# Second weight tile loaded by ScalarE's queue, the first in two parts, three warm-up products in place of four

## The reference

```python
def reference(**kwargs):
    ...
    attn_out = _attn_ref(**attn_kwargs)                 # blocks of 64, a decaying state
    x = ...                                             # 1536 x 512
    x = _moe_ref(x=x, **moe_kwargs)                     # leaky relu between w_in and w_out
    return _moe2_ref(x=x, **moe2_kwargs)

def _moe2_ref(x, w1, w2, w3, w_out):
    a = x @ w1
    b = x @ w2
    h = a * b @ w3
    return (h @ w_out).astype(np.float32)
```

## Time and profile before

| | us |
|---|---|
| median of 3 runs | 512.49 (512.42 to 512.62) |
| the profiled execution | 512.28 |
| its span, first to last instruction | 510.4 |
| TensorE (PE) busy | 505.6 |
| VectorE (DVE) busy | 355.2 |
| ScalarE (ACT) busy | 200.8 |
| GpSimd (POOL) busy | 93.2 |

### The profile page before, as it was taken

One profiled execution on the slowest core, in us unless ns is written; L12 is line 12 of the kernel. 1 busy time (PEld: TensorE's weight loads), 2 busy tenths in 40 slices (PEclk: granted clock), 3 DMA queues, 4 the chain that ended last, 5 costly groups with the idle time before them and its releaser, 6 DMA issues.

```text
span 510.4 us, 9091 instructions
## 1 busy us (share of the span) xinstructions
PE 505.6 (99%) x3568; PEld 417.5 (82%) x3568; DVE 355.2 (70%) x537; ACT 200.8 (39%) x356; POOL 93.2 (18%) x101
## 2 busy tenths in 40 slices
PE   8999999999999999999999999999999999999997
PEld 6888888888888888888888888888888888888886
DVE  4667356767786876877665777697777755878962
ACT  5364243343556433333311546443333214473420
POOL 2223132111122311333300020323333300000000
PEclk9999999999999999999999999999999999999999
DMA  8999582534121111111000031212221116240012
GB/s 278 345 393 334 170 297 85 159 125 127 42 84 42 42 41 42 42 42 41 5 38 0 22 83 34 77 52 88 57 89 63 41 43 205 82 166 0 13 50 103
DMA packets 27065, 51.57 MB, mean 101 GB/s; under 512 B 4232, under 2 KB 4496, under 8 KB 27024
## 3 DMA queue, kind: packets, MB, share of 16 engines
q1 hardware_dynamic: 24560, 43.53, 25.7%
q10 hardware_dynamic: 2432, 7.47, 4.4%
q0 software_dynamic: 32, 0.00, 0.0%
HBM read 45.74 MB, written 5.25 MB: 100 GB/s over the span
## 4 chain that ended last, share of the span: by engine, by line
PE 99%; DVE 0%; issue 0%; DVEq 0%
PE acc L1438 12%; PE acc L1440 11%; PE acc L1439 11%; PE hid L1639 10%; PE hid L1638 10%; PE hid L1637 10%; PE hid L1438 7%; PE hid L1439 7%; PE hid L1440 7%; PE hid L1467 1%; PE hid L1482 1%; PE hid L1495 1%; PE acc L1764 1%; PE acc L1763 1%; PE acc L1765 1%; PE hid L1506 1%
## 5 line engine op out<-in xcount | busy, mean ns | idle before, releaser
L1438 PE MATMUL acc<-g_hi,wb 128*128 128x512 f32 x224 | 87.6, 391 | 0.0
L1439 PE MATMUL acc<-g_lo,wb 128*128 128x512 f32 x224 | 87.2, 389 | 0.0
L1440 PE MATMUL acc<-g_hi,wb 128*128 128x512 f32 x224 | 87.2, 389 | 0.0
L710 POOL TENSOR_TENSOR w_in_lo_place<-stage 128x256 f32<-128x256 f32 x16 | 12.6, 788 | 211.6 <-PE hid L1639 121.7
L1438 PE MATMUL hid<-xy_hi,wa_hi 128*128 128x512 f32 x128 | 50.3, 393 | 0.0
L1440 PE MATMUL hid<-xy_hi,wa_lo 128*128 128x512 f32 x128 | 49.8, 389 | 0.0
L1439 PE MATMUL hid<-xy_lo,wa_hi 128*128 128x512 f32 x128 | 49.8, 389 | 0.0
L1637 PE MATMUL hid<-wa_hi 128*128 128x512 f32 x128 | 49.8, 389 | 0.0
L1638 PE MATMUL hid<-wa_lo,wa_hi 128*128 128x512 f32 x128 | 49.8, 389 | 0.0
L1639 PE MATMUL hid<-wa_hi,wa_lo 128*128 128x512 f32 x128 | 49.8, 389 | 0.0
L1438 PEld LDWEIGHTS acc<-g_hi,wb 128*128 128x128 f32 x224 | 42.0, 188 | 8.9
(11 more groups left out here) (222 smaller groups left out, 931.1 us busy)
## 6 DMA issues: line engine op xcount, KB each, us to landing
stage<-weights SPq DMA_DIRECT2D x109, 256.0 KB, 3.0
w_out_place<-attn ACTq DMA_DIRECT2D x12, 512.0 KB, 4.9
x_hi_place<-attn SPq DMA_DIRECT2D x4, 512.0 KB, 8.9
w_out_place<-attn SPq DMA_DIRECT2D x4, 512.0 KB, 7.8
w_dram<-x_lo_place SPq DMA_DIRECT2D x8, 256.0 KB, 4.4
stage<-w_dram SPq DMA_DIRECT2D x8, 256.0 KB, 2.7
x_lo_place<-attn SPq DMA_DIRECT2D x2, 512.0 KB, 6.5
x_hi_place<-attn ACTq DMA_DIRECT2D x2, 512.0 KB, 6.4
```

Source lines behind the costliest of these rows:

```text
L710: nc.gpsimd.tensor_tensor(s_1, a21, a22, ALU.add).then_inc(s_made, 1)
L1438: nc.tensor.matmul(out, w_hi, a_hi, start=first, stop=False)
L1439: nc.tensor.matmul(out, w_hi, a_lo, start=False, stop=False)
L1440: return nc.tensor.matmul(out, w_lo, a_hi, start=False, stop=final)
```

## The change

The warm-up has three products. SyncE loads the first tile, w3's, in two parts: 128 columns (the left side of the first matmul) with a semaphore of their own, `first_loaded`, then the other 384. The second tile, wl's, is issued by ScalarE before lam's load. ScalarE rounds the first part, then the second tile (both count in `first_hi_done`), then the rest of the first tile, which adds 2 to `hi_done`. TensorE's first matmul waits for `first_hi_done`, its second for `hi_done`. VectorE waits for `first_hi_done` ahead of its first split.

```diff
-WARM_UP = 4
+WARM_UP = 3
...
-            for w in range(8):
+
+            first = source_of(ORDER[0])
+            sp.dma_start(stage[:, STAGED[0], 0:P], weights[first][:, 0:P]).then_inc(first_loaded, 16)
+            sp.dma_start(stage[:, STAGED[0], P:TOK], weights[first][:, P:TOK]).then_inc(staged[STAGED[0]], 16)
+            for w in range(2, 8):
                 load_weight(w)
...
         def _(act):
+            act.dma_start(stage[:, STAGED[1], :], weights[source_of(ORDER[1])]).then_inc(staged[STAGED[1]], 16)
             act.dma_start(pow_row[:, BLOCK:BLOCK + 1], lam).then_inc(lam_loaded, 16)
...
-            w = 0
-            for _ in EARLY_34:
+
+            w3_hi, wl_hi = dest(ORDER[0])[0], dest(ORDER[1])[0]
+            act.wait_ge(first_loaded, 16)
+            nc.scalar.copy(w3_hi[:, 0:P], stage[:, STAGED[0], 0:P]).then_inc(first_hi_done, 1)
+            act.wait_ge(staged[STAGED[1]], 16)
+            nc.scalar.copy(wl_hi, stage[:, STAGED[1], :]).then_inc(first_hi_done, 1)
+            act.wait_ge(staged[STAGED[0]], 16)
+            nc.scalar.copy(w3_hi[:, P:TOK], stage[:, STAGED[0], P:TOK]).then_inc(hi_done, 2)
+            w = 2
+            for _ in EARLY_34[2:]:
                 weight_hi(w)
                 w += 1
...
+            dve.wait_ge(first_hi_done, 2)
             for w in range(len(EARLY_34)):
                 weight_lo(w)
...
-            pe.wait_ge(hi_done, max(PLACE["w3", 0], PLACE["wl", 0]) + 1)
+            pe.wait_ge(first_hi_done, 2)
             for slot, cols in enumerate(first_step):
+                if slot == 1:
+                    pe.wait_ge(hi_done, max(PLACE["w3", 0], PLACE["wl", 0]) + 1)
                 nc.tensor.matmul(w34_acc[slot], w3(0)[0][:, cols], wl(0)[0], start=True, stop=False)
```

More of the change, by code:

```diff
@@ L450, in build @@
         lam_loaded = sem("lam_loaded")
+        first_loaded = sem("first_loaded")
+        first_hi_done = sem("first_hi_done")
         pow_chain = sem("pow_chain")
```

## The result

| | before | after |
|---|---|---|
| median, us (lowest to highest) | 512.42 (511.91 to 512.79, 8 runs) | 513.88 (513.09 to 515.13, 8 runs) |
| ratio | | 1.0032 [1.0022, 1.0041] |
| the profiled execution, and its span | 512.28, 510.4 | 514.16, 512.4 |

A forecast was written before the change was run, and what follows sets the result against it. TensorE, busy 505.6 of 510.4 us, was taken as the bound. An earlier start of 0.41 us was worth 0.21, so the median of 512.49 less 0.21 gave 512.28 us, range 511.9 to 512.9.

The forecast's parts named there:

- What bounds the kernel: Whole span: TensorE is the bound, busy 505.6 of 510.4 us, with hardly any waits.
- the three ways in which an edit can change the time: TensorE's stream: its length, the moment from which useful instructions run, and the pace at which they run.
- Second tile, split of the first, warm-up: Start: second tile lands at 3.86, the first product starts at 4.57, 0.41 us sooner; its second instruction finds its data.
- What 0.41 us are worth: TensorE's first products: with the pace rising at 6.56 as before, half of the earlier start, 0.21 us, is gained.
- the rise hardly wanders: TensorE's early pace: argument against a later rise, as four earlier times lie within 0.34 us.
- The next limit: Second tile pair: its weights need VectorE's split of the fourth tile, leaving 0.39 us of room; 0.21 fits.
- What is later, and hidden: Splits, weight loads and lam's powers: delays, lam's 0.45 to 0.58 us against 1.8 of room, are off the path.
- VectorE's new wait: VectorE's first split: starts near 5.1 us, ready at 5.85 for TensorE's need at 6.45, so hidden.
- Clock later: Rival, TensorE's start: fewer warm-ups and a dry array delay the pace's rise, up to 513.7 us; chance 0.09.
- A landing: Rival, early loads: second or fourth tile lands late and cancels the gain, 512.5 to 512.8 us; chance 0.23.
- Slower: Outcome for the whole kernel: slower by over 0.2%, through a pace rise delayed by 2.6 us or more; chance 0.07.

The follow-up runs named there:

- no_wait: The changed kernel without VectorE's added wait, all three roundings counting in `hi_done`: 513.08 us, ratio 1.0013.
- pad_dve: The kernel before with two long-met waits added to VectorE's program after its first 14 splits: 513.38 us, ratio 1.0022.
- swapped kernels: Changed kernel without VectorE's wait; ScalarE issues lam, then the 128 columns; SyncE issues the second tile first, rounded first; four or three warm-ups: 512.32, 512.40 us.
- swapped4: The one of the swapped kernels with four warm-up products: 512.32 us, ratio 0.9997.
- no_wait_lam: Changed kernel without VectorE's added wait, with four warm-ups and lam issued by SyncE between the first tile's two parts: 513.21 us, ratio 1.0016.
- lam_sp_pad: Changed kernel with eight long-met waits added on ScalarE and lam issued by SyncE ahead of the first tile's parts: 513.60 us, ratio 1.0034.
- pow_late: The kernel before, with GpSimd waiting for the second tile's landing before it makes the powers: 512.94 us, ratio 1.0013.
- lam_late: The kernel before, with ScalarE issuing lam's load after its first rounding: 514.18 us, ratio 1.0033.
- after_warm4: The changed kernel with four warm-up products: 514.09 us, ratio 1.0040.

## Why the prediction was wrong, step by step

*"What bounds the kernel", and the three ways in which an edit can change the time: the step that cost most.* The list lacked a fourth: what follows TensorE's last instruction. The tail, with its last landing of 1.7 us, was put at no change without a row for it, since the diff touches only the first us. It grew by 1.1 us in the trace, and by 0.8 to 0.95 by the medians of no_wait and pad_dve.

*Second tile, split of the first, warm-up.* Right in the main. The tile was issued at 0.75; ScalarE took up its rounding at 3.91, with landing at 3.86 predicted; the roundings took 0.30 and 0.51; the first product started at 4.58 for 4.57, and the second instruction found its data. The first tile's part of 128 columns landed 2.9 us after its issue, at 3.65, outside the bounds of 2.45 to 3.55; it did no harm, as the second tile came later still. The 4.57 has a slip of 0.03: with the lengths of the kernel before (4.30 to 4.98) a landing at 3.86 gives 4.54. And the 0.41 us were counted from the latest of seven starts, 4.63 to 4.98, against 4.53 to 4.81 in the eight traces with parts and the early second tile, so that the usual gain is nearer to 0.3.

*What 0.41 us are worth, and "the rise hardly wanders".* The sum of 0.21 took the rise at 6.56 as a constant, from one trace and from four times that lie within 0.34 us. Over the traces it wanders by 3 us between executions with an equally full start. The change did not move it: 7.0 and 4.7 in the two traces of after. A gain of 0.21 is hard to see beside that, and the swapped kernels show none (the trace of swapped4 has also the wait of 0.54 for the fourth tile). The Trainium skill (TensorE: Matmul & The Clock Gate, What's actually happening) does say that the number of slow products varies from run to run of one kernel; these traces agree, and I had not used it.

*The next limit.* In its place, though mis-sized: the second pair waited 0.32 us for VectorE's split of the fourth tile, which was rounded from 7.60. The third and fourth tiles were "issued where they were", but the landings moved. In the next trace of after the pair started at 7.78, so this term wanders as well. The trace of swapped4 has the wait again (0.54), and those of no_wait_lam (0.57) and lam_sp_pad (0.33).

*"What is later, and hidden": the other step that failed.* lam was priced by the delay of its issue, 0.45 to 0.58 us, against 1.8 us of room. It lost 1.8 us in landing (2.17 to 3.95), landing with the large tile ahead of it, and 1.4 more as GpSimd's six operations then ran beside VectorE's splits (3.70 us for 2.34). The Trainium skill (SBUF — State Buffer, SBUF: two separate sides) says that a VectorE operation with two inputs in SBUF and a GpSimd operation that reads SBUF lock each other out; the traces agree, as far as the six operations took 2.3 to 2.9 us where the operations were through before or soon after the first split, and 3.5 to 4.7 where they lay beside splits. The sum is 3.2 us. It did not show where I had put it: GpSimd's decay of the keys started at 17.47 for 17.17, as other things hold it too, and TensorE had no wait there. The mistake was to follow lam to the keys alone and not through SyncE, which stands waiting for the store of the powers with all later weight loads behind it. pow_late prices this step at 0.5 us. And the stretch from the second pair to 65 us is 0.2 to 1.1 us longer than with powers on time in eight of the nine traces with late powers beside lam_late's (2.5 there).

*VectorE's new wait.* It was told as a start at 5.1 for VectorE, which is right and hidden. That it is one more instruction, and that the code packet stands elsewhere half a millisecond later, was in no step. It is this wait that makes the tail longer: without it, in no_wait, the landing takes 1.8 us again.

*Sum of what was measured.* 0.5 and 0.8 to 0.95 make 1.3 to 1.45 of the 1.46 us. That this fits so well is in part luck: the 95% intervals are 0.15 to 1.1 us for pow_late and 0.7 to 1.6 for pad_dve, and the gain at the start and the wait for the fourth tile have no price of their own.

*The rivals.* "Clock later" gave 513.7, near the 513.88 measured, and would have been right for the wrong reason: neither after_warm4 nor the traces of after bear it out. Such a late rise was seen, in three traces where the array was dry for 0.5 us or more. "A landing" named the wait of TensorE for the fourth tile, which came. "Slower" as a whole had 0.07, because neither of the two costs, powers and tail, was among the cases, and the range ended at 512.9 for the same reason.

*What stays open.* Why TensorE waits 0.2 to 0.8 us with "issue" near 95 us in every trace (0.5 here, 0.3 in the earlier trace rows); which transfer holds lam; and whether the small packet itself delays the report of the landing. The two coincide in the seven traces with 2.9 us, and in the second trace of after, with 2.1, the cost was 0.25. So that an instruction more on VectorE lengthens the tail is shown, by pad_dve and no_wait; that it does so through the packet is argued, not shown.

## What to carry to other kernels

A small load that a long chain hangs on is best issued ahead of the large ones, and where it is moved back it is priced by the landing of what is ahead of it, then followed through everything that waits in order behind its last step. A test of an edit of a few tenths of a us needs a control that adds the same number of instructions and nothing else, as two waits of no use cost 0.95 us here. And a start that is sooner by 0.3 us can't be measured beside a rise of the pace that wanders by ten times that.

## What the hardware showed

- Two waits on VectorE that were long met cost 0.95 us of 512. In the trace the last output's landing took 2.9 us for 1.8, with a packet of 8 KB of an instruction queue right behind the outputs' last bytes. The same on ScalarE cost nothing.
- The rise of TensorE's pace from 0.43 to 0.23 us came anywhere between 4.4 and 7.5 us from the span's start, in seventeen traces with at most 0.4 us without work before the first product. In three traces with 0.5 to 0.7 us without work there it came at 8.8 to 10.2; other executions of one of these kernels were not slow.
- A load of lam issued at 0.76 lands at 2.2; issued at 1.19 behind a 256 KB tile, or at 1.20 behind a 64 KB part with such a tile on the other queue, it lands at 3.9 to 4.4.
- Two 256 KB tiles issued at 0.75 from two queues landed at 4.25 and 4.46; issued one behind the other on one queue, they landed at 3.55 and 4.30.
- Six small operations of GpSimd took 2.3 us alone and up to 4.7 beside VectorE's splits.
